# Expert loop of a fused attention, FFN and routed-expert kernel: hidden-unit transposes after the first up chunk, ids product after tile 1's up products

## The reference, cut to what matters

```python
h = np.maximum(x[b, s] @ w1[e], 0.0)      # 512 -> 1024
out[b, s] = p[e] * (h @ w2[e])            # 1024 -> 512
```

## Time and profile before

| what | value |
|---|---|
| median of 3 runs | 935.76 us (933.89 to 935.84) |
| profiled execution | 933.35 us |
| its span in the trace | 931.5 us |
| PE busy | 898.2 us, 96% |
| DVE / ACT / POOL busy | 324.1 / 250.2 / 147.2 us |

### The profile page before, as it was taken

The page is one execution under the profiler, slowest core; times in us unless marked ns, Lnnn a source line. Parts: engine busy times, 40 slices in busy tenths (PEclk is TensorE's granted clock), DMA queues, the critical chain, the costliest instruction groups (busy, mean ns, idle before and its releaser), DMA issues.

```text
span 931.5 us, 18920 instructions
## 1 busy us (share of the span) xinstructions
PE 898.2 (96%) x7112; PEld 788.9 (85%) x7113; DVE 324.1 (35%) x612; ACT 250.2 (27%) x497; POOL 147.2 (16%) x150
## 2 busy tenths in 40 slices
PE   5999999889999999999999999999999999999996
PEld 5999999679999999889988999999877777787774
DVE  4566676421221112122123323211565252332221
ACT  3566766411111111011101111111225342332221
POOL 0211122329000000000000000034332221122111
PEclk9999999979999999999999999999999999999998
DMA  5544442103000000000000000022118151311111
GB/s 130 122 129 108 124 124 73 59 24 114 1 18 18 1 0 35 0 1 34 1 1 1 35 1 12 35 93 88 46 46 304 42 217 39 116 58 34 39 34 40
DMA packets 41884, 55.84 MB, mean 60 GB/s; under 512 B 24944, under 2 KB 25072, under 8 KB 41840
## 3 DMA queue, kind: packets, MB, share of 16 engines
q1 hardware_dynamic: 38320, 44.66, 15.6%
q0 software_dynamic: 3360, 10.49, 3.5%
q10 hardware_dynamic: 160, 0.07, 0.0%
HBM read 45.76 MB, written 9.96 MB: 60 GB/s over the span
## 4 chain that ended last, share of the span: by engine, by line
PE 90%; DVE 3%; issue 3%; ACT 1%; DMA 1%; SPq 0%; ACTq 0%; DVEq 0%; POOL 0%; POOLq 0%
PE bank L1415 22%; PE bank L1417 21%; PE bank L1416 21%; PE bank L1347 7%; PE bank L1363 4%; PE bank L1320 4%; PE bank L1460 2%; PE bank L1588 2%; PE bank L1331 2%; PE bank L1478 2%; PE bank L1483 1%; PE bank L1308 1%; PE bank L1540 1%; DMA rows<-in_moe_w 1%; ACT W L831 1%
## 5 line engine op out<-in xcount | busy, mean ns | idle before, releaser
L957 DVE SCALAR_TENSOR_TENSOR hid_lo<-bank,hid_hi 128x384 fp32r<-128x384 f32 x96 | 53.6, 558 | 320.7 <-ACT hid_hi L806 320.7
L806 ACT ACTIVATE hid_hi<-bank 128x384 fp32r<-128x384 f32 x96 | 47.2, 492 | 375.8 <-PE bank L1417 375.8
L1415 PE MATMUL bank<-uT_hi,W 128*128 128x384 f32 x384 | 130.9, 341 | 1.2 <-DVE uT_lo L974 1.2
L1417 PE MATMUL bank<-uT_hi,W 128*128 128x384 f32 x384 | 130.7, 340 | 0.0
L1416 PE MATMUL bank<-uT_lo,W 128*128 128x384 f32 x384 | 130.2, 339 | 0.0
L1415 PE MATMUL bank<-W,hid_hi 128*128 128x512 f32 x288 | 117.3, 407 | 0.0
L1417 PE MATMUL bank<-W,hid_lo 128*128 128x512 f32 x288 | 115.1, 400 | 0.0
L1416 PE MATMUL bank<-W,hid_hi 128*128 128x512 f32 x288 | 114.3, 397 | 0.0
L1347 PE MATMUL bank<-vv,kp 64*128 64x65 f32 x1152 | 78.2, 284 | 3.0 <-DVE rows L931 3.0
L1415 PEld LDWEIGHTS bank<-uT_hi,W 128*128 128x128 f32 x384 | 73.5, 192 | 5.4 <-DVE uT_lo L974 1.5
L1347 PEld LDWEIGHTS bank<-vv,kp 64*128 64x128 f32 x1152 | 75.3, 202 | 3.2 <-issue 3.2
(11 more groups left out here) (229 smaller groups left out, 1305.4 us busy)
## 6 DMA issues: line engine op xcount, KB each, us to landing
rows<-in_moe_w SPq DMA_DIRECT2D x16, 1024.0 KB, 6.6
stage<-in_moe_w_ch SPq DMA_DIRECT2D x16, 512.0 KB, 4.1
qk_raw<-in_q SPq DMA_DIRECT2D x32, 144.0 KB, 2.9
qk_raw<-in_k SPq DMA_DIRECT2D x32, 144.0 KB, 3.0
vv<-in_v SPq DMA_DIRECT2D x32, 144.0 KB, 3.1
x_rows<-rows SPq DMA_DIRECT2D x6, 768.0 KB
out<-stage,oid_now POOLq DMA_INDIRECT x20, 2.8
u_pair<-in_moe_U SPq DMA_DIRECT2D x4, 72.0 KB, 4.4
```

Source lines behind the costliest of these rows:

```text
L806: act.activation(hid_hi[:, n % 2], bank[:, HB[n % 2], 0:TOK], ACT.Relu).then_inc(hid_hi_out, 1)
L957: dve.scalar_tensor_tensor(out=hid_lo[:, n % 2], in0=bank[:, HB[n % 2], 0:TOK], scalar=0.0, in1=hid_hi[:, n % 2].bitcast(F32), op0=ALU.max ...
L1415: pe.matmul(dst, lhs_hi, rhs_hi, start=start, stop=False)
L1417: return pe.matmul(dst, lhs_lo, rhs_hi, start=False, stop=stop)
```

## The change

Three edits on PE's stream. In every tile the transposes of half 0 come after the first chunk of half 1's up product (3 matmuls) instead of the second (6 matmuls). Tile 1 uses the same function `up_rest`, and with it the ids product is issued after all up products of tile 1, instead of after the transposes, with two chunks behind it. No instruction is added or removed, and no other engine's stream is touched.

```diff
             def up_rest(i, par):
-                up_part(par, 1, range(KC // 2))
+                up_part(par, 1, range(1))
                 turn_h(i, 0)
-                up_part(par, 1, range(KC // 2, KC))
+                up_part(par, 1, range(1, KC))
...
             up_start(1, 0, 0)
-            up_part(0, 1, range(KC // 2))
-            turn_h(1, 0)
+            up_rest(1, 0)
             pe.wait_ge(oh_ab_ready, 1)
             for c in range(C):
...
             mm.then_inc(r_pe, 1)
-            up_part(0, 1, range(KC // 2, KC))
             down_start(1, 0, 0)
             turn_h(1, 1)
```

## The result

The changed kernel takes 930.53 us (median of 18 runs), the kernel before 933.99 us in its 18 runs. The ratio is 0.9962 with a 95% interval of 0.9951 to 0.9974: 0.38% or 3.5 us faster. The forecast was 0.7 us faster and 935.1 us, with a range from 932.8. Its base, the median of the first three runs, lay 1.8 us above the median of all 18; the effect itself was five times what I gave it. The direction, the places and the waits were as forecast, their price was not: the rival "fast hand-off", to which I had given 0.20, had 3.7 us faster.

A forecast was written before the change was run, and what follows sets the result against it. PE, busy 96% of the span, was taken as the bound. Fourteen loop tiles at 0.09 us gave -1.3, tile 1 +0.6, sum -0.7 us: 935.76 - 0.7 = 935.1 us, range 932.8 to 937.1.

The forecast's parts named there:

- fast hand-off: Rival: in loop tiles the relu's release takes 0.05 us and the transposes restart free; 3.7 us faster, 932.1 us; chance 0.20.
- the price of the new wait: Loop tile, transposes waiting for the relu: 0.17 us release plus 0.10 restart, leaving a gain of 0.09 us a tile.
- L: Time from the end of half 0's relu to the transposes' weight load in a loop tile, taken as 0.17 us.
- s: Restart cost of the transposes after PE stalls on the relu in a loop tile, taken as 0.10 us.
- One of my signs of being wrong: Transposes' weight load in the changed profile: a relu wait shorter than 0.10 us would show the forecast wrong.
- The dear end: Loop tiles, relu wait dearer than the one it replaces: release 0.25 us as DVE's, 938.4 us; rival's chance 0.13.
- The page that was weighed: Trainium skill page: semaphore read in 50 to 100 ns, so the relu wait in loop tiles gives 0.16 to 0.21 us each.
- The three tiles at nothing: Tiles 3, 6 and 11: DVE reaches the low part late, splitting the next expert's weights, so they gain nothing.
- Tile 1: Ids product behind nine up products: down product at 683.71 instead of 683.15, a loss of 0.56 us, ends 0.3 and 0.9.
- no pause before the second transposes: Half 1's transposes: relu ends at 788.73, six down products put the load at 789.07, leaving 0.34 us and no stall.
- R: End of half 0's relu in a tile, the zero point from which the prediction counted the down product's start.
- One sign: Loop tiles: the first down product should start 0.09 us earlier after the relu's end than before.

The follow-up runs named there:

- one_more_instruction: The changed kernel with one semaphore-increment instruction on PE between the wait for the relu and the transposes; one run, tile 0 to 19 distance 245.81 us against 244.95.
- split_wait_six: The kernel before, old order, but only the third product of a chunk waits for DVE's low part, the first two for ACT's high part; 924.29 us, ratio 0.9901.

## Why the prediction was wrong

**The step that failed** is the price of the new wait, "I take L = 0.17, the nearest row" and "I take 0.10" for the restart. L was 0.05 and s 0.06, together 0.11 instead of 0.27, so a tile gained 0.24 us on the mean of the 14 instead of 0.09. That is 3.4 us instead of 1.3, 2.1 of the 2.8 that the forecast of the effect lacked. I had called 0.17 a bound and then used it as a value. One of my signs of being wrong, a relu wait shorter than 0.10, came true. Tile 3's load was not released at 707.56: it started with the matmul ahead of it, as an unstalled load does, and the row says only that ACT had been done before. The row that measured a release was the one at 193.32, 0.05 us, which I made an end of the gain and the rival "fast hand-off". one_more_instruction shows why its neighbour had 0.12.

**The dear end** came from DVE's 0.25. Tile 3 of split_wait_six shows a release by DVE in 0.05. In the old order the down product has a second wait and, in the loop, an address instruction between the wait and the load. The records of PE's sequencer, which the timeline leaves out, show both in the trace of before. In tile 9 the low part ends at 787.67, the semaphore instruction (L1572) starts at 787.71, the register instruction for the address at 787.82 and the load at 787.91, and 15 of the 17 loop tiles have the same distances (the other two are 0.05 us longer). In tiles 1 and 2, where addresses are fixed, only the first stands there and the load comes 0.12 us after the low part. No kernel was run with the address instruction ahead of the wait and the wait as it was.

**The page that was weighed** had it nearer. The load followed the relu by 0.05 us. That is the lower end of the 50 to 100 ns which the Trainium skill, "Advanced Engine Details and Errata", section Network/Comms, gives for a sequencer's read of a semaphore. The gain by it was an estimated 0.16 to 0.21 a tile, and 0.24 was measured. The 0.12 of the attention stage lay above the page's range, and the instruction behind the wait accounts for that.

**The three tiles at nothing** (3, 6 and 11) gained 0.10 to 0.11 each. DVE is late in them, as said, but its lateness counts from work of the tile before, which follows that tile's down products, and these no longer carry a restart of 0.10: DVE's first weight split in tile 6 starts 7.13 us after tile 5's down product before, and 7.02 after. With tile 2's 0.03 that is 0.34 us that the sum left out.

**Tile 1** lost 0.21 us where 0.56 was forecast. Release and restart together were 0.11 there too, where I had 0.22; the 18 small products took 0.64 us to their very end (I gave 0.81, from a row of wider ones), and DVE followed in 0.04 instead of 0.11. Together 0.35. (Counted in starts, PE stood there for about 1.7 us, against 1.5 before; the "about 1.9 in pieces" of the prediction was too high, and no sum used it.)

**What held.** The wait for the low part vanished but for tiles 1, 3, 6 and 11; the relu's wait came in every tile but tile 0, which has another product in between; there was no pause before the second transposes (their load 0.33 to 0.36 after the relu of half 1, 0.34 forecast); the down product's place, R + 2.51 + L + s with 0.23 more or less for each product more or less behind the transposes, fitted the kernels with two, three and four products ahead to 0.01. The ids product's delay reached nothing behind it: tile 3, which waits for the weights, stepped 14.28 us against 14.39. The arithmetic of cover was right, and with the true 0.11 it gives 0.25 us a tile. One sign did not follow from it: by its own terms the down product would have started at R + 2.78, not 0.09 us ahead of the old 2.77, since 0.10 of the old cost lay behind that start. It started at 2.62.

**The range** hung on the wrong base as well: 935.76 was the median of three runs of a kernel that later spread from 931.5 to 936.6, and on the right one its lower end would have been 933.99 - 0.7 - 2.3 = 931.0, still above 930.5.

## What to carry to other kernels

Count a stall in matmul starts, not in the idle column: a pause that the column gave as 0.21 us cost 0.48, and one of a weight load that it gave as 0.43 cost 0.23. Compare lines of waits only with lines of the same engine. A release that the trace does not show is priced from a row in which the engine was really released, not from one in which it was merely ready. Before moving work to cover a wait, look whether all of the waiting work needs what it waits for: here the first two of three products did not.

## What the runs showed of the hardware that I had not expected

- PE followed ACT, and DVE too, in 0.05 us when nothing stood between the wait and the weight load; one sequencer instruction there added 0.06 to 0.07 us (0.11 to 0.12 in tiles 1 to 19 of one_more_instruction), a semaphore and a register instruction together 0.19 to 0.20 (tile 9 of before).
- Four fp32 transposes from rest cost 0.06 us more than in a stream (tile 10 of the changed kernel), a 128x128x512 product 0.10 (0.08 in tiles 1 and 2).
- A weight load came 0.17 us late at no cost: with the transposes after four products it waited 0.20 us and started 0.06 us ahead of its matmul instead of 0.23, and the matmuls kept their distance of 0.23.
